# Tile 0's gelu in place in PSUM over three pairs, an earlier second half of the values, and x2 ahead of the table load

## The reference

```python
kv_pool = kv.reshape(B, H//4, 4, W//4, 4, C).mean(axis=(2, 4))      # 384x32 pixels -> 768 keys, C = 128
k = v = kv_pool.reshape(B, -1, C) @ w_sr
s = (q @ k.T) / sqrt(C); a = softmax(s)                             # q: 12288 rows
x = (a @ v).reshape(12288, 128)
h = x @ w_in1;  x = (h * sigmoid(1.702 * h)) @ w_out1               # 128 -> 2048 -> 128
h = x @ w_in2;  y = (h * clip(h + 3, 0, 6) / 6) @ w_out2
```

## Time and profile before

| | |
|---|---|
| time, median of 3 runs | 1301.45 us (1301.41 to 1301.69) |
| the profiled execution's own time | 1301.61 us |
| its span | 1299.9 us |
| busy share of PE, DVE, ACT, POOL | 98%, 80%, 79%, 3% |
| granted TensorE clock, mean | 1.00 |

### The profile page before, as it was taken

How to read it: one execution, slowest core, us unless ns; L and a number is a source line. 1 busy time by engine, 2 the same in 40 slices (tenths; PEclk the granted TensorE clock), 3 DMA queues, 4 the chain that set the end, 5 groups by cost and what they waited for, 6 DMA issues and landing times.

```text
span 1299.9 us, 18319 instructions
## 1 busy us (share of the span) xinstructions
PE 1276.5 (98%) x5782; PEld 1064.2 (82%) x5782; DVE 1037.7 (80%) x1071; ACT 1031.8 (79%) x1209; POOL 42.9 (3%) x47
## 2 busy tenths in 40 slices
PE   6889999999999999999999999999999999999998
PEld 6768888888888888888888888888888888888786
DVE  3788888878888888788888887888888888877667
ACT  2778888778888888888888888888888788887676
POOL 1820000000000000000000000000000000000000
PEclk9999999999999999999999999999999999999999
DMA  9321303213123032131230321312303213022000
GB/s 306 93 46 37 74 0 73 48 24 73 27 46 73 0 73 48 24 73 25 48 73 0 73 48 24 73 23 49 73 0 73 48 24 73 21 43 66 1 9 17
DMA packets 183621, 65.67 MB, mean 51 GB/s; under 512 B 104497, under 2 KB 176305, under 8 KB 183345
## 3 DMA queue, kind: packets, MB, share of 16 engines
q1 hardware_dynamic: 182544, 65.29, 22.3%
q10 hardware_dynamic: 1056, 0.13, 0.1%
HBM read 22.87 MB, written 6.34 MB: 22 GB/s over the span
## 4 chain that ended last, share of the span: by engine, by line
PE 96%; DVE 2%; ACT 1%; DMA 1%; issue 0%; SPq 0%; DVEq 0%; ACTq 0%
PE pair L877 16%; PE pair L878 16%; PE pair L879 16%; PE bank_av L877 9%; PE bank_av L879 9%; PE bank_av L878 9%; PE bank_out L878 6%; PE bank_out L877 6%; PE bank_out L879 6%; PE pair L886 1%; DMA kv_sb<-in_kv_dram 1%; DVE p_low L704 0%; DVE p_turned L694 0%; DVE mid_lo L737 0%; ACT work L513 0%
## 5 line engine op out<-in xcount | busy, mean ns | idle before, releaser
L753 DVE TENSOR_TENSOR mid_lo<-work,mid_hi 128x1024 fp32r<-128x1024 f32 (+1 forms) x193 | 235.0, 1218 | 134.9 <-ACT mid_hi L526 134.7
L877 PE MATMUL pair<-x_hi,w_hi 128*128 128x512 f32 x768 | 302.1, 393 | 3.1 <-DVE x_lo L726 1.4
L878 PE MATMUL pair<-x_lo,w_hi 128*128 128x512 f32 x768 | 299.5, 390 | 0.0
L879 PE MATMUL pair<-x_hi,w_lo 128*128 128x512 f32 x768 | 299.0, 389 | 0.0
L498 ACT ACTIVATE work<-pair 128x1024 f32<-128x1024 f32 x192 | 197.2, 1027 | 124.0 <-PE pair L879 121.6
L737 DVE TENSOR_TENSOR mid_lo<-work,mid_hi 128x1024 fp32r<-128x1024 f32 x192 | 235.8, 1228 | 28.6 <-ACT mid_hi L505 28.6
L746 DVE SCALAR_TENSOR_TENSOR work<-work,pair 128x1024 f32<-128x1024 f32 (+1 forms) x193 | 232.4, 1205 | 4.0 <-ACT work L513 3.6
L513 ACT ACTIVATE work<-pair,half 128x1024 f32<-128x1024 f32 (+1 forms) x193 | 212.1, 1100 | 5.0 <-PE pair L879 4.9
L505 ACT ACTIVATE mid_hi<-work 128x1024 fp32r<-128x1024 f32 x192 | 202.6, 1055 | 4.7 <-PE bank_av L879 2.5
L526 ACT ACTIVATE mid_hi<-work 128x1024 fp32r<-128x1024 f32 (+1 forms) x193 | 201.5, 1044 | 1.8 <-DVE work L746 1.7
L877 PEld LDWEIGHTS pair<-x_hi,w_hi 128*128 128x128 f32 x768 | 144.1, 188 | 41.8 <-ACT work L498 7.1
(11 more groups left out here) (132 smaller groups left out, 1523.1 us busy)
## 6 DMA issues: line engine op xcount, KB each, us to landing
p_keys<-p_turned SPq DMA_DIRECT2D x368, 96.0 KB, 2.2
out_dram<-y_sb SPq DMA_DIRECT2D x94, 64.0 KB, 2.5
inv_b<-inv_dram SPq DMA_DIRECT2D x23, 256.0 KB, 3.3
q_raw<-in_q_dram SPq DMA_DIRECT2D x88, 64.0 KB, 2.1
kv_sb<-in_kv_dram SPq DMA_DIRECT2D x6, 768.0 KB, 9.8
w_raw<-in_moe_w_in_dram SPq DMA_DIRECT2D x2, 1024.0 KB, 13.8
kv_sb<-in_kv_dram SPq DMA_DIRECT2D x6, 256.0 KB, 8.9
inv_dram<-inv_t SPq DMA_DIRECT2D x92, 0.5 KB
```

Source lines behind the costliest of these rows:

```text
L753: dve.tensor_tensor(mid_lo[mid2(t, p)][:, part], act2[p % 2][:, part], mid_hi[mid2(t, p)][:, part], ALU.subtract).then_inc(mid2_ready, 1)
L877: pe.matmul(dst, a_hi, b_hi, start=start, stop=False)
L878: pe.matmul(dst, a_hi, b_lo, start=False, stop=False)
L879: return pe.matmul(dst, a_lo, b_hi, start=False, stop=stop)
```

## The change: orders on four engines, three PSUM places, and tile 0's gelu

1. The SP queue waits for the last kv row before it issues the weights.
2. The second half of the values is computed right after the last part of the keys, in `bank_out`, instead of after two of the second score halves in `bank_av`; q of tile 1 is transposed into `bank_av` instead of a half of `pair[2]`, and after the first second-half score. On ACT `v_hi_copy(1)` moves ahead of `q1_copy` and the first exponential; on DVE `v_lo_part(1)` moves ahead of `maximum(0, 1)`. q of tile 0 is transposed earlier, and the pixel additions and pooled rows are spread differently between the other work.
3. In tile 0 alone, gelu writes its result back into the PSUM pair it read, and both parts are split from there. The pairs rotate over all three (1, 2, 0), and PE waits for `mid1_ready` (the low part is done) instead of `act1_ready` (gelu is done) before it writes a pair again.
4. `inverse(1)` on DVE moves behind the second `act1_lo`.
5. After tile 0, ACT copies x2's high part before it loads the table of Exp, and DVE does x2's low part and the first maximum before the last `p_lo`.

```diff
         def hidden1_in(t, p):
-            return pair[1 - p % 2] if isinstance(t, int) and t == 0 else pair[2]
+            return pair[(1, 2, 0)[p % 3]] if isinstance(t, int) and t == 0 else pair[2]
+
+        def activated1(t, p):
+
+            return hidden1_in(t, p)[:, :] if isinstance(t, int) and t == 0 else act1[p % 2]
...
-        VALUES_IN = [pair[2][:, 0:HALF], bank_av[:, 0:HALF]]
-        Q_FIRST_IN = [bank_out[:, :], pair[2][:, 512:1024]]
+        VALUES_IN = [pair[2][:, 0:HALF], bank_out[:, 0:HALF]]
+        Q_FIRST_IN = [bank_out[:, :], bank_av[:, :]]
...
+            sp.wait_ge(kv_row_loaded[ROW_GROUPS - 1][KV_ROWS - 1], 16)
             load_weights(0, w_in1)
...
-                if later(n - 1):
+                if later(t):
                     act.wait_ge(mid1_ready, n - 1)
-                act.activation(act1[p % 2], hidden1_in(t, p)[:, :], ACT.Gelu_apprx_sigmoid).then_inc(act1_ready, 1)
+                act.activation(activated1(t, p), hidden1_in(t, p)[:, :], ACT.Gelu_apprx_sigmoid).then_inc(act1_ready, 1)
...
-                act.activation(mid_hi[p % 2][:, :], act1[p % 2], ACT.Copy).then_inc(mid1_hi_ready, 1)
+                act.activation(mid_hi[p % 2][:, :], activated1(t, p), ACT.Copy).then_inc(mid1_hi_ready, 1)
...
             pooled_copy(0)
             k_hi_copy(0)
+            q_high_first()
             v_hi_copy(0)
-            q_high_first()
...
+            v_hi_copy(1)
             q1_copy()
             exponential(0, 0)
-            v_hi_copy(1)
             exponential(0, 1)
...
+            x2_high(0)
             load_table(ACT.Exp)
-            x2_high(0)
...
-                dve.tensor_tensor(mid_lo[p % 2][:, :], act1[p % 2], mid_hi[p % 2][:, :],
+                dve.tensor_tensor(mid_lo[p % 2][:, :], activated1(t, p), mid_hi[p % 2][:, :],
                                   ALU.subtract).then_inc(mid1_ready, 1)
...
                 maximum(0, s)
-                if s == 1:
+                if s == 0:
                     v_lo_part(1)
...
-            inverse(1)
 
             for p in range(PAIRS):
                 act1_lo(0, p)
+                if p == 1:
+                    inverse(1)
...
-            for n in range(P_PARTS):
+            for n in range(P_PARTS - 1):
                 p_lo(1, n)
             x2_low(0)
-            for s in range(SLOTS):
+            maximum(2, 0)
+            p_lo(1, P_PARTS - 1)
+            for s in range(1, SLOTS):
                 maximum(2, s)
...
-                    if p == 1:
-                        pe.wait_ge(exp_ready, SLOTS + 3)
-                    elif p > 1:
-                        pe.wait_ge(act1_ready, p - 1)
+                    if p in (1, 2):
+                        pe.wait_ge(exp_ready, SLOTS + 1 + p)
+                    elif p > 2:
+                        pe.wait_ge(mid1_ready, p - 2)
...
                 else:
-                    pe.wait_ge(act1_ready, PAIRS)
+                    pe.wait_ge(mid1_ready, PAIRS)
                 scores(i + 2, 0)
-                pe.wait_ge(act1_ready, PAIRS * (i + 1))
+                if later(i):
+                    pe.wait_ge(act1_ready, PAIRS * (i + 1))
```

More of the change, by code:

```diff
@@ L764, in _ @@
             k_lo_part(0)
-            for a in range(KV_ROWS):
-                add_row_pixels(KV_GROUPS - 2, a)
+            add_row_pixels(KV_GROUPS - 2, 0)
+            add_row_pixels(KV_GROUPS - 2, 1)
+            q_low_first()
+            add_row_pixels(KV_GROUPS - 2, 2)
+            add_row_pixels(KV_GROUPS - 1, 0)
             v_lo_part(0)
-            q_low_first()
-            for a in range(KV_ROWS):
-                add_row_pixels(KV_GROUPS - 1, a)
+            add_row_pixels(KV_GROUPS - 1, 1)
+            add_row_pixels(KV_GROUPS - 1, 2)
             k_lo_part(1)
@@ L984, in _ @@
             keys_of(0)
+            turn_q_first(0)
             pool_group(5)
@@ L987, in _ @@
             pool_loaded_row(6, 0)
-            turn_q_first(0)
             pool_loaded_row(6, 1)
-            pool_loaded_row(6, 2)
-            pool_loaded_row(7, 0)
-            keys_of(1)
             pe.wait_ge(k_lo_ready, 1)
@@ L996, in _ @@
             scores_half(0, 0, 0)
+            pool_loaded_row(6, 2)
+            scores_half(0, 1, 0)
+            pool_loaded_row(7, 0)
+            keys_of(1)
             pool_loaded_row(7, 1)
-            scores_half(0, 1, 0)
-            pool_loaded_row(7, 2)
             pe.wait_ge(v_lo_ready, 1)
             scores_half(0, 2, 0)
+            pool_loaded_row(7, 2)
             keys_of(2)
-            turn_q_first(1)
+            values_of(1)
             pe.wait_ge(k_lo_ready, PARTS)
             scores_half(0, 0, 1).then_inc(scores_ready, 1)
+            turn_q_first(1)
             scores_half(0, 1, 1).then_inc(scores_ready, 1)
-            values_of(1)
-            pe.wait_ge(q1_copied, 1)
             scores_half(0, 2, 1).then_inc(scores_ready, 1)
             pe.wait_ge(v_lo_ready, 2)
+            pe.wait_ge(q1_copied, 1)
             scores(0, 3)
```

## The result

| | before | after |
|---|---|---|
| time, median of 15 runs each | 1301.51 us (1301.06 to 1302.54) | 1298.51 us (1297.55 to 1299.67) |
| after / before | | 0.9976, 95% interval 0.9969 to 0.9982 |
| the profiled execution's own time | 1301.61 us | 1299.67 us |
| its span | 1299.9 us | 1297.9 us |

What follows compares the result with a forecast made beforehand. PE, 96% of the chain, bounds the kernel, so only its idle time in the first 90 us can go: 1.4 + 0.8 + 0.3 + 0.7 = 3.2 us, from 1301.45 to 1298.25, say 1298.3 us; range 1297.3 to 1299.8.

Steps and rivals of the forecast that it cites:

- Part 1: At the start, up to tile 1's first scores: computing the values' second half earlier saves 1.4 us, bounds 0.5 and 2.0.
- all is 1.4 earlier: At the beginning of tile 0's first layer: everything there starts 1.4 us earlier.
- The SP wait: Weights issued after the last kv row: first matrix lands at about 30 us, costing nothing up to about 34.
- First project: Tile 0's first project: inverse behind the second low part and a low part of 1.22 us save 0.8 more.
- End of the layer: Tile 0's last project: last high part starts when project1(0,5) is done, PE waits about 1.1 us; 0.3 saved.
- x2, −0.7: Before tile 1's weighted values: x2's parts moved ahead remove PE's whole wait of 0.72 us.
- at the old price: Two p_lo on DVE after tile 0, from 69.8 to 73.1 us, were taken at 1.66 us each.
- Gelu in PSUM: Tile 0's first layer: gelu into PSUM takes 1.03 to 1.06 us, low parts out of it 1.22.
- Part 1 paid more, not less: Rival at the start: the earlier values save only 0.5 to 0.8 us instead of 1.4, time 1299.1; chance 0.19.
- Gelu was not slow: Rival in tile 0: gelu into PSUM takes 2.05 us, nothing is left of the gain, time 1301.5; chance 0.04.
- bring the slow rate back: Rival at the start: new pauses return PE to its slow rate, adding 4.7 us, time 1303.0; chance 0.03.

Runs made afterwards that it cites:

- v_hi behind the exponential: The changed kernel with v_hi_copy(1) on ACT moved back behind tile 1's q copy and the first exponential; 1299.06 us, one run.
- ACT shifted: The changed kernel with six empty semaphore increments added at ACT's start; 1297.38 us, one run.
- orders alone: The changed kernel with tile 0's gelu back in SBUF and two pairs as in the kernel before, keeping only the orders; 1298.36 us.
- no SP wait: The changed kernel without SP's wait for the last kv row before the weights; 1297.92 us.

## Why the prediction was right, and where its reasons were not

- **Part 1, −1.4.** Measured −1.5 at T1, with the marks where they were said to be (keys −0.6 for −0.5, `both_banks` −2.1 for −2.0, then 0.6 given back). v_hi's place in ACT's queue is the cause (v_hi behind the exponential). That "all is 1.4 earlier" behind it holds only with the later parts; alone they lost 1.0 of it again.
- **The SP wait, 0.** Right. The weights landed at 29.1, where I took 30.
- **First project, −0.8.** Measured −0.9, but I gave all of it to `inverse` and to the low part's price without saying that the two overlap. The place alone is 0.33 once the source is PSUM. The rest is the low part no longer running into POOL, which either edit achieves: `inverse` held the low part back into a split.
- **End of the layer, −0.3.** Failed: 0.0. The step said that the last high part starts when `project1(0,5)` is done. It did so 0.32 later than its neighbours do after theirs, because of the stall on ACT; with the list shifted the 0.3 is there (P0 to P7 in 17.70 instead of 18.01). My 1.1 for the wait before the last project was 1.39 for the same reason (1.06 with the list shifted).
- **x2, −0.7.** The size is right (−0.9), the step is not. It kept p_lo "at the old price" of 1.66 beside POOL, but POOL, undisturbed by DVE, was done by 67.6. So the low part would have been in time in either order. The order would have been enough too, with gelu in SBUF.
- **Gelu in PSUM.** Its prices were right (1.01 to 1.02 for 1.03 to 1.06; 1.23 for 1.22), and the rule of the Trainium skill (SBUF — State Buffer, "Who interferes with whom") on two SBUF inputs held in both directions: low parts out of PSUM are all 1.23 and POOL's subtractions 1.3, those out of SBUF go up to 2.15 (2.35 in before) and POOL's to 2.28. The 0.06 us by which I estimated a low part out of PSUM to be dearer doesn't show: 1.23 there, 1.22 for after's p_lo, which are of the same size, read two SBUF operands and start when POOL is done. What I didn't ask is whether PE waits for the long ones. In the middle of the layer it doesn't, so this part, which looks like the main one, brings only about 0.3 us at the last low part beyond the orders, and with the stall nothing.
- **The rivals.** Part 1 paid more, not less. Gelu was not slow. The new pauses of 0.82 and 0.69 did not bring the slow rate back: the clock record that begins at 18.06 us holds 1.00 for 1280 us, and behind the pauses the matmuls come every 0.17 and 0.23 us, as in before. My reading of the earlier trace rows, a granted clock of 1.00 in the slow stretch too, was wrong: in all fourteen traces the first clock record begins within 0.1 us of the first matmul at the fast rate. A slow stretch at half the rate would fit a clock of 1.2 GHz, but no record covers it.

**From 3.3 at W to 3.0 in time.** The lead at the last matmul is 2.5 us in after's trace, 3.0 in its second profile, 3.4 in "orders alone". From one tile's weighted values to the next's takes 52.07 us in most passes of before's trace and never 52.13; in after's trace eleven passes take 52.13, in its second profile six, in "orders alone" none. So two executions of one kernel differ in this; whether the change has a part in it is not shown, since before has one trace. Why some passes are longer stays open.

## What to carry to other kernels

Before crediting an edit, ask whether another edit of the same change already removes the wait: here two pairs of edits each covered the same one (`inverse` and PSUM, x2's order and PSUM), and only kernels with both undone show what either is worth. A lead won early is kept only if the work behind it does not slide into another engine's traffic, so a part that is worth 1.5 us in company can be worth nothing alone. And where a stage ends in a wait for one pair, splitting the first and the last pair and giving the buffers more depth can be worth more than a faster middle: 2.4 us here, against about 0.3 for gelu in PSUM.

## What the hardware showed that I had not expected

- **A stall at a place in an engine's instruction list.** In after, ACT's high part at 68.20 starts 0.32 us later than the semaphores allow, and six empty instructions put ahead move this to another high part. Instruction traffic of 8 KB on queue 14 is seen at 68.86, 0.66 us behind the late start, and in "ACT shifted" at 62.36, 0.93 behind; two other such packets of after, at 59.50 and 60.73, stand beside no late start. The Trainium skill (Runtime: NRT & Kernel Launch, "Instruction fetch mechanics") says that an engine's list is refilled in blocks and that crossing a boundary is mostly hidden. That fits a stall tied to a position; if it is the cause, it was not hidden here and cost the 0.3 us. That the fetch is the cause was not shown.
- **Contention lengthens both sides, and outlasts itself.** With gelu in SBUF, POOL's subtractions beside DVE's low parts take 2.04 instead of 1.29, and its last one starts 8.7 us later than in after, counted from the keys (73.67 less 18.33, against 66.30 less 19.62). So DVE's first two p_lo, which would run alone, suffer too (1.9 each instead of 1.2).
- **ACT into PSUM is no slower.** Gelu of 128x1024 back into the pair it read takes 1.01 to 1.02 us, against 1.01 to 1.03 into SBUF, and the copy out of PSUM 1.03 against 1.06 out of SBUF. The Trainium skill (ScalarE: Activation LUTs, "Step-by-step: what each stage is for") calls PSUM the faster destination; the trace agrees by 0.01 us in the mean of tile 0's eight (1.01 against 1.02) and by 0.02 for a gelu that starts after idle time; for one right behind another ACT instruction it is the other way round (1.02 against 1.01).
- **The start varies.** Fourteen traces have PE's first fast pooling matmul between 14.4 and 18.1 us and the first keys matmul between 18.00 and 19.62. The two do not go strictly together: "no SP wait" is fast from 14.5 us, but PE then waits for pixel additions on late kv groups and begins the keys at 18.99. Between after's two profiles the keys differ by 1.15 of the 1.6 us in time. Why the fast rate begins so differently stays open.
